# Router of chunks 0 to 4: rows of y through DRAM, 32x32 block turns on the vector engine, and one set of logits per chunk in four column groups

## The reference

```python
scores = scale * np.matmul(q, k.transpose(0, 1, 3, 2))      # 4 batches, 8 heads, 576 x 64
attn_out = np.matmul(scores * Dmat[None], v)                # Dmat[h, i, j] = gamma_h ** (i - j), 0 above
x = attn_out as (2304, 512)
gate = 1.0 / (1.0 + np.exp(-(x @ w_gate)))                  # 512 -> 1536
y = (gate * (x @ w_val)) @ w_out                            # 1536 -> 512
logits = y @ r_gate                                         # 512 -> 8: the router
noisy_logits = logits + np.log1p(np.exp(y @ r_noise)) * noise
top2 = the two largest of 8; top2_w = softmax over the two
out[t] = sum over the two experts e of top2_w * (np.maximum(y[t] @ w1[e], 0.0) @ w2[e])
```

## Time and profile before

| | |
|---|---|
| median of 3 runs | 1016.32 us (1015.77 to 1018.06) |
| profiled execution | 1016.23 us; span on the core 1014.4 us |
| PE busy | 991.9 us, 98% of the span |
| DVE, ACT, POOL busy | 39%, 33%, 18% |
| TensorE clock, mean of the span | 0.996 |
| DMA | 119.5 MB, 118 GB/s in the mean |
| DMA share by 25 us slices from 100 us | 3, 8, 9, 5, 2, then 0 or 2 up to 480 us (tenths) |

### The profile page before, as it was taken

The page is one execution under the profiler, slowest core; times in us unless marked ns, Lnnn a source line. Parts: engine busy times, 40 slices in busy tenths (PEclk is TensorE's granted clock), DMA queues, the critical chain, the costliest instruction groups (busy, mean ns, idle before and its releaser), DMA issues.

```text
span 1014.4 us, 15342 instructions
## 1 busy us (share of the span) xinstructions
PE 991.9 (98%) x6108; PEld 915.7 (90%) x6108; DVE 393.6 (39%) x956; ACT 333.7 (33%) x572; POOL 182.0 (18%) x162
## 2 busy tenths in 40 slices
PE   6999999999999999999999999999999999999995
PEld 5888989999998998998998999899898989898994
DVE  4455331411410420330334566627272645536320
ACT  1332332521512512511423443434243434343320
POOL 2765440010020020020020311110102021111202
PEclk9999999999999999999999999999999999999998
DMA  8986389520020020020028178274635546351403
GB/s 292 346 264 194 131 264 282 191 85 1 0 94 0 0 94 0 0 94 0 1 71 272 65 136 239 62 206 96 197 66 141 129 114 156 104 135 22 115 12 42
DMA packets 75081, 119.50 MB, mean 118 GB/s; under 512 B 14160, under 2 KB 43216, under 8 KB 73872
## 3 DMA queue, kind: packets, MB, share of 16 engines
q1 hardware_dynamic: 60160, 79.23, 25.6%
q0 software_dynamic: 12560, 35.55, 15.0%
q10 hardware_dynamic: 2304, 3.93, 1.0%
HBM read 89.78 MB, written 41.59 MB: 130 GB/s over the span
## 4 chain that ended last, share of the span: by engine, by line
PE 96%; SPq 1%; DMA 1%; issue 0%; POOLq 0%; ACT 0%; DVE 0%; ACTq 0%
PE bank L525 30%; PE bank L527 29%; PE bank L526 29%; PE bank L537 1%; PE bank L603 1%; PE bank L573 1%; PE bank L582 1%; DMA kv_in<-vn 1%; PE bank L558 1%; PE bank L595 1%; PE bank L575 1%; DMA result<-y_out,idx 0%; SPq L386 0%; SPq L378 0%; SPq L380 0%
## 5 line engine op out<-in xcount | busy, mean ns | idle before, releaser
L525 PE MATMUL bank<-x_hi,w_sb 128*128 128x384 f32 x576 | 195.4, 339 | 0.2 <-DVE x_lo L1034 0.2
L527 PE MATMUL bank<-x_hi,w_sb 128*128 128x384 f32 x576 | 192.7, 335 | 0.0
L526 PE MATMUL bank<-x_lo,w_sb 128*128 128x384 f32 x576 | 192.6, 334 | 0.0
L1476 POOL DMA_INDIRECT result<-y_out,idx x40 | 65.3, 1631 | 362.8 <-ACT y_out L944 244.4
L1034 DVE TENSOR_TENSOR h_raw<-bank,sig 128x384 f32<-128x384 f32 x64 | 35.7, 558 | 241.3 <-PE bank L527 241.3
L1460 POOL DMA_INDIRECT rows_scratch<-yt,slot_i x36 | 38.6, 1072 | 396.1 <-DVE slot_i L1142 386.9
L525 PEld LDWEIGHTS bank<-x_hi,w_sb 128*128 128x128 f32 x576 | 108.2, 188 | 1.2 <-issue 0.3
L526 PEld LDWEIGHTS bank<-x_lo,w_sb 128*128 128x128 f32 x576 | 108.2, 188 | 0.2
L527 PEld LDWEIGHTS bank<-x_hi,w_sb 128*128 128x128 f32 x576 | 108.1, 188 | 0.0
L525 PE MATMUL bank<-wo_hi,h_hi 128*128 128x512 f32 x216 | 86.5, 400 | 0.0
L525 PE MATMUL bank<-xa_hi,w_hi 128*128 128x384 f32 x256 | 85.8, 335 | 0.0
(11 more groups left out here) (156 smaller groups left out, 1794.1 us busy)
## 6 DMA issues: line engine op xcount, KB each, us to landing
w_in<-w SPq DMA_DIRECT2D x8, 2048.0 KB, 9.3
w_raw<-w SPq DMA_DIRECT2D x32, 512.0 KB, 7.4
rows_scratch<-pads POOLq DMA_DIRECT2D x8, 1290.0 KB, 26.4
xa_in<-rows_scratch SPq DMA_DIRECT2D x32, 192.0 KB, 6.7
result<-zeros POOLq DMA_DIRECT2D x1, 4864.0 KB, 51.6
qk_in<-qT SPq DMA_DIRECT2D x16, 288.0 KB, 3.6
qk_in<-kT SPq DMA_DIRECT2D x16, 288.0 KB, 4.5
kv_in<-kn SPq DMA_DIRECT2D x16, 256.0 KB, 4.8
```

The source lines that it names most:

```text
L525: pe.matmul(o, a_hi, b_hi, start=first, stop=False)
L526: pe.matmul(o, a_hi, b_lo, start=False, stop=False)
L527: return pe.matmul(o, a_lo, b_hi, start=False, stop=last)
L1476: pool.indirect_dma_start(out, bass.IndirectOffsetOnAxis(ap=idx[:, n:n + 1], axis=0), y_out[n % 3][:, :], None, compute_op=ALU.add,).then_ ...
```

## The change

For chunks 0 to 4 PE no longer turns y. SP stores `yt[:, j]` to a DRAM scratch (`y_rows`) when ACT has copied tile j, and loads it back in four DMAs of 32 partitions, tiles 0 and 1 together (1024 runs of 512 bytes), tile 2 apart (512 runs). DVE turns each tile by a 32x32 block transpose ahead of its work for block f = 2 of the next chunk's MLP. PE makes the logits of all three tiles at once behind block f = 2: 16 float32 matmuls with the router's columns (padded to 32) as weights and 96 columns of `y_turned`, each into one of four groups of 32 PSUM partitions. DVE copies the result and turns it. The router's steps and `positions` stand one block later. The last chunk keeps the old way. Four pairs of small DMAs (32 x 4 x 8 words) load the router's columns in a second layout, between the loads of attention units 7 and 8. `y_in` and `y_turned` lie over the last four blocks of `h_hi` and `h_lo`, and the loads of y wait for y_ready of the whole chunk.

```diff
+            for b in range(P // Q):
+                for i, r in enumerate((r_gate, r_noise)):
+                    sp.dma_start(wr_by4[Q * b:Q * b + Q, :, E * i:E * i + E],
+                                 r[:, b, :].rearrange("(j k) e -> j k e", k=KB)).then_inc(wr_by4_in, 16)
...
+            def store_y(j):
+                sp.dma_start(y_rows[P * j:P * j + P, :], yt[:, j, 0:D]).then_inc(y_stored, 16)
+
+            def load_y(first, end, landed):
+                for b in range(P // Q):
+                    sp.dma_start(y_in[Q * b:Q * b + Q, first:end, :, :].rearrange("i j a d -> i (j a) d"),
+                                 y_rows[P * first:P * end, P * b:P * b + P].rearrange("(a i) d -> i a d", i=Q)
+                                 ).then_inc(landed, 16)
+
             with sp.Fori(1, NCH) as c:
                 sp.wait_ge(val_ready, FB * c)
                 load_x(c)
+                for j in range(2):
+                    sp.wait_ge(y_copied, TJ * c + (j + 1 - TJ))
+                    store_y(j)
+                sp.wait_ge(y_ready, TJ * c)
+                sp.wait_ge(y_stored, 16 * TJ * c - 16)
+                load_y(0, 2, y01_in)
+                sp.wait_ge(y_copied, TJ * c)
+                store_y(2)
+                sp.wait_ge(y_stored, 16 * TJ * c)
+                load_y(2, TJ, y2_in)
...
+            def chunk_logits(c):
+                pe.wait_ge(y_turned_ready, TJ * c + TJ)
+                for k in range(KB):
+                    for a in range(P // Q):
+                        mm = pe.matmul(LG[Q * a:Q * a + Q, 0:TJ * Q].rearrange("p (j i) -> p j i", i=Q), wr_by4[:, k, :],
+                                       y_turned[:, :, a, Q * k:Q * k + Q], start=(k == 0), stop=(k == KB - 1),
+                                       skip_group_check=True)
+                mm.then_inc(logit_ready, 1)
...
-                    if f == 0:
-                        turn_y(prev, 2)
-                    if f == 1:
-                        logits(prev, 2)
-                    if f == 6:
+                    if f == 2:
+                        chunk_logits(prev)
+                    if f == 7:
                         positions(prev)
...
-                        if j and f == 3:
+                        if last and j and f == 3:
                             turn_y(c, j - 1)
-                        if j and f == 9:
+                        if last and j and f == 9:
                             logits(c, j - 1)
...
                 for k in (2 * j, 2 * j + 1):
                     act.wait_ge(scattered[k], 16 * c)
+                act.wait_ge(y_stored, 16 * TJ * c)
                 act.wait_ge(y_ready, TJ * c + j + 1)
...
+            def turn_y(c):
+                for j in range(TJ):
+                    if j == 0:
+                        dve.wait_ge(y01_in, 16 * P // Q * (c + 1))
+                    if j == 2:
+                        dve.wait_ge(y2_in, 16 * P // Q * (c + 1))
+                    dve.transpose(by_feature(y_turned[:, j, :, :]), interleaved(y_in[:, j, :, :])
+                                  ).then_inc(y_turned_ready, 1)
...
+                    else:
+                        dve.wait_ge(logit_ready, c + 1)
+                        link(dve.tensor_copy(lgT[:, :], bank[6][:, 0:TJ * Q]))
+                        link(dve.transpose(lg[:, :, :].rearrange("p j e -> p (j e)"), lgT[:, :]))
...
                 for f in range(FB):
+                    if f == 2:
+                        turn_y(prev)
                     dve.wait_ge(sig_ready, FB * c + f + 1)
...
-                    if 2 <= f < 8:
-                        router(prev, f - 2, at)
+                    if 3 <= f < 9:
+                        router(prev, f - 3, at)
```

More of the change, by code:

```diff
@@ L85, in program @@
         rows = nc.dram_tensor("rows_scratch", (E * REGION, ROW), F32, kind="Internal").ap()
+        y_rows = nc.dram_tensor("y_rows_scratch", (CH, D), F32, kind="Internal").ap()
         def sem(name):
@@ L147, in program @@
         yt = b_top.place("yt", [P, TJ, ROW])
-        yT = b_top.place("yT", [P, KB, P])
+        zeros = b_top.place("zeros", [P, P])
+        lgT = b_top.place("lgT", [P, TJ * Q])
+        lg = b_top.place("lg", [P, TJ, Q])
+        wr_by4 = b_top.place("wr_by4", [P, KB, Q])
+        tail_of_h = (FB - 4) * CH * 4
+        y_in = Region(160 * KIB + tail_of_h, 6 * KIB).place("y_in", [P, TJ, P // Q, P])
+        y_turned = Region(178 * KIB + tail_of_h, 6 * KIB).place("y_turned", [P, TJ, P // Q, P])
         sm = keep
         gap = Region(1536, 512)
-        zeros = Region(3584, 512).place("zeros", [P, P])
-        lg = sm.place("lg", [P, TJ, 2 * E])
         absz = sm.place("absz", [P, TJ, E])
@@ L178, in program @@
         meta_in = [c.place(f"meta_in{i}", [P, TE, ROW - D]) for i in range(2)]
+        yT = c.place("yT", [P, KB, P])
         wtab = c.place("wtab", [P, TILES + 1])
@@ L221, in program @@
         x_dma = sem("x_dma")
+        wr_by4_in = sem("wr_by4_in")
+        y_stored = sem("y_stored")
+        y01_in = sem("y01_in")
+        y2_in = sem("y2_in")
         zeroed = sem("zeroed")
@@ L259, in program @@
         y_copied = sem("y_copied")
+        y_turned_ready = sem("y_turned_ready")
         yT_ready = sem("yT_ready")
@@ L312, in program @@
         over_done = sem("over_done")
-        LINKS = 19
+        LINKS = 20
         COUNT = 4 * 2 * E + TJ * E
@@ L584, in back @@
                 mm.then_inc(attn_ready, 1)
-            GATE, VAL, Y, YT, ROUTE = bank[0:2], bank[2:4], bank[4:6], bank[6], bank[7]
+            GATE, VAL, Y, YT, LG, ROUTE = bank[0:2], bank[2:4], bank[4:6], bank[6], bank[6], bank[7]
             POS = 4 * 2 * E
             ident = cst[:, C_ID:C_ID + P]
+            def chunk_logits(c):
[6 more added lines that the diff above has]
+                mm.then_inc(logit_ready, 1)
             def turn_y(c, j):
                 pe.wait_ge(y_copied, TJ * c + j + 1)
-                pe.wait_ge(yT_copied, TJ * c + j)
+                pe.wait_ge(yT_copied, j)
                 for k in range(KB):
@@ L598, in logits @@
             def logits(c, j):
-                pe.wait_ge(yT_copied, TJ * c + j + 1)
+                pe.wait_ge(yT_copied, j + 1)
                 if j == 0:
@@ L707, in _ @@
             pe.wait_ge(const_in["cst"], 16)
+            pe.wait_ge(wr_by4_in, 16 * 2 * P // Q)
             output(0, first=True)
@@ L757, in counts @@
             def counts():
-                pe.wait_ge(router_step, LINKS * NCH)
+                pe.wait_ge(router_step, LINKS * NCH - 1)
                 pe.matmul(ROUTE[:, COUNT:COUNT + E], cst[:, C_ONE:C_ONE + P], msum[:, 0, :], start=True, stop=True
@@ L845, in yT_copy @@
             def yT_copy(c, j):
-                act.wait_ge(logit_ready, TJ * c + j)
-                act.wait_ge(yT_ready, TJ * c + j + 1)
+                act.wait_ge(logit_ready, NCH - 1 + j)
+                act.wait_ge(yT_ready, j + 1)
                 act.copy(yT[:, :, :].rearrange("p k t -> p (k t)"), bank[6][:, :]).then_inc(yT_copied, 1)
@@ L883, in mlp @@
                         h_round(c, f - 1)
[L884 to L887, removed]
+                    if 4 <= f < 7:
+                        router(prev, f - 4)
                 h_round(c, FB - 1)
@@ L892, in output @@
                 y_copy(c, 0)
-                yT_copy(c, 0)
+                if last:
+                    yT_copy(c, 0)
                 if not last:
@@ L902, in output @@
                     xt_round(0, 0)
-                yT_copy(c, 1)
                 if last:
+                    yT_copy(c, 1)
                     xt_round(0, 1)
@@ L1075, in h_rest, with router @@
                 tt(h_lo[:, f, :], h_raw[:, f, :], h_hi[:, f, :].bitcast(F32), ALU.subtract).then_inc(h_lo_ready, 1)
-            def router(c, step, at, er=cst[:, C_ER:C_ER + E]):
+            def turn_y(c):
[6 more added lines that the diff above has]
+                                  ).then_inc(y_turned_ready, 1)
+            def router(c, step, at, er=cst[:, C_ER:C_ER + E], last=False):
                 def link(ins):
@@ L1085, in router @@
                 if step == 0:
-                    dve.wait_ge(logit_ready, TJ * c + TJ)
-                    link(dve.tensor_copy(lg[:, :, :].rearrange("p j e -> p (j e)"), bank[7][:, 0:TJ * 2 * E]))
+                    if last:
+                        dve.wait_ge(logit_ready, NCH - 1 + TJ)
+                        link(dve.tensor_copy(lg[:, :, 0:2 * E], bank[7][:, 0:TJ * 2 * E].rearrange("p (j e) -> p j e", j=TJ)))
+                    else:
+                        dve.wait_ge(logit_ready, c + 1)
+                        link(dve.tensor_copy(lgT[:, :], bank[6][:, 0:TJ * Q]))
+                        link(dve.transpose(lg[:, :, :].rearrange("p j e -> p (j e)"), lgT[:, :]))
                     dve.scalar_tensor_tensor(out=absz[:, :, :], in0=z, scalar=-1.0, in1=z, op0=ALU.mult, op1=ALU.max
@@ L1146, in router @@
                     link(tt(msum[:, 0, :], msum[:, 2, :], picked[:, 2, :], ALU.add))
```

(13 more changed lines are left out.)

## The result

The changed kernel takes 1027.97 us (median of 4 runs, 1026.55 to 1030.45), the kernel before on the same chip 1016.12 us: a ratio of 1.0117, with a 95% interval from 1.0105 to 1.0130. It is slower by 11.9 us. The profiled execution took 1030.45 us and is the longest of the four; its span is 1028.6 us, 14.2 more than before.

What follows compares the result with a forecast made beforehand. PE, holding 96% of the chain, was taken to bound the kernel. From 1016.2 us: 20.7 less for removed work, plus 7.0 logits, 0.4 quiet chunks, 23 chunk 0's wait, 2 clock: 1027.9 us, range 1009 to 1037.

Steps and rivals of the forecast that it cites:

- What leaves PE, 20.7 us: Turns, logits and extra block time leave PE's program: 4.14 us per chunk, 20.7 us saved over five chunks.
- The logits, 1.4 us a set plus 0.1 of DVE's tail: PE's 16 new matmuls cost 7.0 us over five chunks; waiting for DVE adds 0.4 us over chunks 1 to 4.
- a floor of 0.038 us a record: In the logits, column groups overlap only down to about 0.038 us a matmul record; 32 records take at least 1.2 us.
- change of mode: Extra 0.1 us added to each set of logits matmuls on PE, beside 32 records at 0.04 us.
- Quiet chunks: In chunks 1 to 4 DMAs land in time, with 0.2 to 2 us left; PE waits 0.1 us each for DVE.
- The small loads on SP: Eight added issues delay attention unit 8's load from 41.99 to about 46 us, before PE's need at 56.91; cost nothing.
- Chunk 0, 23 us: PE waits 23 us (16 to 28) for chunk 0's turned y, whose DMAs run beside POOL's pad rows and zeroes.
- its 128 packets are through by 161: Chunk 0's store of tile 1 doesn't delay the first loads; ACT's copy of tile 2 starts at 160.2 us (T0).
- start and landing of the two legs: At chunk 0, two successive round trips of y cost 8 us (4 to 13) beside their packets.
- One packet for one packet: Beside POOL's fill, each packet of y pays for one of POOL's, whatever its size; 62 packets per us taken.
- Rival 1: At chunk 0 several small y packets pass per POOL packet: wait 5 us, 1009 us in all; chance 12%.
- The clock, 2 us: Behind PE's wait at chunk 0 the clock runs at half rate, costing 2 us (0 to 4).

Runs made afterwards that it cites:

- e5: e1 with a second, unused set of the 16 logits matmuls in the same four column groups; 0.65 us a set, single run.
- e7: e1 with the logits one block later on PE (behind block 3), positions and router steps also one later; 1000.05 us.
- e1: Changed kernel with POOL's pad rows issued after chunk 0's second loads of y landed, zeroes behind chunk 1's scatter; 1000.32 us, ratio 0.9837 to the kernel before.
- e9: Changed kernel with y's loads in 2 KB rows, 128 packets a tile instead of 512, stores unchanged, logits wrong; only PE's wait read, 12.9 us against 24.6.
- e8: Changed kernel with 130 unused matmuls on PE ahead of the wait for chunk 0's turned y; 1024.15 us, ratio 1.0076.
- e6: e1 with a second, unused set of 16 logits matmuls, all in one group of 32 partitions; 2.62 us a set, single run.

## Why the prediction was right

The forecast of 1027.9 us for the measured 1027.97 is closer than its terms deserve. Point by point:

- **What leaves PE, 20.7 us.** The tiles stand 8.16 us apart and blocks 0 and 1 cost 4.16: as forecast.
- **The logits, 1.4 us a set plus 0.1 of DVE's tail.** 1.08 us in all. I kept a floor of 0.038 us a record from 64-column groups; the four groups reach 0.020 (e5). What a visit costs beyond the set, my "change of mode", is 0.37 instead of the 0.1 that I gave it. Over five chunks the forecast was 2 us too dear: this term was mis-sized.
- **Quiet chunks.** No wait for DMA, and 0.06 us for DVE (e7): the third transpose ends just when PE arrives, as worked out.
- **The small loads on SP.** They cost nothing: PE is as late ahead of them as behind them.
- **Chunk 0, 23 us.** 24.6 us, and e1 shows that the fill makes all of it. But one step in it was wrong: "its 128 packets are through by 161". The store of tile 1 was issued at 155.99, its first packets came at about 160.4, 4.4 us later, its last at about 164, and it landed at 165.89, 3.1 us behind T0. The forecast put that at nothing. It put 8 us on start and landing of the two legs, which were 9.8, and 27 on their packets, which were 22.9: the rate was 70 per us and not 62, and the fill ran dry in the second loads. So this term is near by luck too: 3.1 and 1.8 too little, 4.1 too much.
- **One packet for one packet.** 700 against 699 in the trace, and e9 halves the wait with the same bytes. Rival 1 is out: neither the counts nor a wait of 24.6 us allow several of y's packets for one of q0's.
- **The clock, 2 us.** 2.4 by the rows of the changed kernel, 2.2 by e8.

Too dear by 2 on the logits, too cheap by 1.6 on the wait and 0.4 on the clock: they cancel. The mechanism held, a wait at chunk 0 alone, packet against packet, with the clock behind it; the floor of the logits did not, and that the number is met within 0.1 us is luck.

## What to carry to other kernels

Before you put a DMA on the way to the bounding engine, look at the queue records of every place where it will run, not of the mean chunk: a loop of five that is fine in four can lose in one what all five gain. Beside a saturating transfer, count packets, not bytes, and count a start and a landing for each leg that must wait for the one before, at the price that they have beside that transfer: a start was 4.4 us here instead of 0.9. If the fill has slack and the new transfer has none, move the fill: that turned 1.2% slower into 1.6% faster.

## What the hardware showed beyond expectation

- A store of 256 KB takes 2.4 us to land with the queues free and 9.9 us beside the fill (e1 and the changed kernel). Its packets moved for some 3.6 us of that (160.4 to 164); 4.4 us passed before the first and 1.9 behind the last. No run shows what the 4.4 us are spent on.
- In the list of waits 0.3 us per chunk stood against DVE, of which DVE caused 0.06 (e7).
- The attention's start differs from run to run in what does not differ in code: the first copy of y was at 142.84 us in e7 and 148.35 in e6. The clock goes with it: 10.2 us at 0.50 from 31.9 us on in e6, none in the first 60 us of e7.
